# One more round of expert work in the first pass: the first expert starts on one tile in plain f32, the second on two

## The chip, the cores and the metric

The kernel runs on one core of a Trainium2 chip. The metric is the device time of one execution in microseconds (us). All times below come from one profiled execution of the kernel or from its timed runs.

## The reference

Three stages follow one another: attention that keeps only the 32 largest scores of each row, a mixture of eight experts whose gates are balanced by eight rounds of row and column normalisation, and a dense two-layer network. There are 2 x 576 = 1152 tokens of width 512.

```python
scores = scale * np.matmul(q, k.transpose(0, 1, 3, 2))          # q, k, v: (2, 8, 576, 64)
mask = scores >= kth                                             # the 32 largest of 576 stay
attn = exp(scores - max) * mask / (sum + 1e-9)
x = (attn @ v) as (1152, 512)

P = np.exp(x @ w_gate - max)                                     # (1152, 8)
for _ in range(8):
    P /= P.sum(1, keepdims=True) + 1e-09
    P /= P.sum(0, keepdims=True) + 1e-09
    P *= N / E
for e in range(8):                                               # w1[e]: (512, 1024), w2[e]: (1024, 512)
    out += P[:, e:e + 1] * (np.maximum(x @ w1[e], 0.0) @ w2[e])

h = out @ w_in                                                   # (512, 2048)
g = h * np.tanh(log1p(exp(h)))
return g @ w_out                                                 # (2048, 512)
```

## The kernel before, in words

**Tiles and chunks.** The 1152 tokens are nine tiles of 128. An expert's 1024 hidden columns are eight chunks of 128, numbered `f`. A chunk has an up part (`up`, line 622: weights stationary, tokens moving) and a down part (`down`, line 637: hidden tile stationary, 512 columns of weights moving). Both run in the split form: weights, tokens and hidden values are each a high and a low half of type f32r, and three products (high by high, high by low, low by high) replace one. An up part is 4 x 3 matmuls whose columns are the tokens. A down part is three matmuls of 512 columns for each tile. A tile and an expert together are the unit of work here: 9 x 8 = 72 such pairs must be done.

**Splitting.** For every chunk SP loads 2 x 256 KB of weights into one of four slots of `w_raw` (`load_slot`, lines 389 and 390), ScalarE copies them to `w_hi` (`split_hi`, line 898 through `copy`) and GpSimd subtracts to get `w_lo` (`split_lo`, line 1501). SP loads a slot again when `w_lo_done` says that GpSimd has read it. For hidden values ScalarE writes `h_f` and `ha_hi` (lines 970, 971) and GpSimd `ha_lo` (line 1508).

**Attention.** Nine tiles `T` of eight heads `h`. For each head TensorE transposes the masked probabilities of the head four back (line 514, and line 518 for the rest of a pair), computes the scores (504), and for every second head multiplies by the values in plain f32 (528, 533). VectorE finds the 32 largest scores in pairs of heads (1190, 1192), and masks from tile 3 on. In tiles 0 and 1 GpSimd masks (1532, 1535), in tile 2 it masks every second head. The next tile's queries are loaded by `next_queries` (381, 382), copied by ScalarE (`queries_high`, at the fourth head of the tile before), lowered by GpSimd and transposed by TensorE (493). A finished tile of attention is scaled with `row_sums` on VectorE (1199, 1201), transposed by `x_transposed` (541), and copied to `x_f`, `x_hi`, `x_lo`.

**First pass (`a`).** One expert chunk is put behind each head, `LAG = 5` heads into a tile. It begins at head 5 of tile 2. Its rounds are: expert 0 for tiles 0 and 1, experts 1 to 7 for tiles 0 to 2, and, as a ninth round, expert 0 again for tiles 2 to 4. So its 72 chunks hold 2 + 21 + 3 = 26 pairs. Results of the experts 0 to 6 go to DRAM (`spill`) and come back later; the last two are added by `add_last_a` (lines 1337 and 1341) while the second pass is on its first expert. Logits and the normalisation of the gates run between chunks behind attention.

**Second pass (`bc`).** For each expert the tiles that are left: expert 0 the tiles 5 to 8, the others the tiles 3 to 8, so 4 + 42 = 46 pairs. Its hidden values are copied high by ScalarE and low by VectorE (1302, 1311) out of PSUM. Expert 0 has one unit of 512 columns in each chunk with two banks in turn, the others two units of 384. The wait that frees a bank asks for the low half two units back:

```python
pe.wait_ge(hb_lo, units_bc(e, f) + j - 1 + TWO)
```

In program order TensorE does `up(f + 1)` before `down(f)`. The last stage (lines 846, 868) is the dense network; in its first half a chunk is two units of 320 columns and five tiles.

**Orders written by hand.** Each engine's order is fixed. On SP the queries of tile 2 are asked for before the first eight weight loads, which wait until all keys have left `w_raw`. On GpSimd each `chunk_a` is a `hidden_low` followed by the split of the chunk two ahead:

```python
chunk_a(*chunk_at(2, 7))
mask(2, 5)
chunk_a(*chunk_at(3, 0))
chunk_a(*chunk_at(3, 1))
mask(2, 7)
```

Of the kernel before, what the change touches and what calls it, by code (L numbers as in the profile page):

```python
# [11 lines left out]
def build(nc, q, k, v, w_gate, w1, w2, w_in, w_out, spill, out):  # L12
# [12 lines left out]
    DM = H * D  # L25
# [32 lines left out]
    NA = E + 1  # L58
    FIRST = 2
    LAST_UP = FIRST + BLK  # L60
    REST_BC = NT - LAST_UP

    def part_a(e):

        if isinstance(e, int) and e == 0:
            return 0, FIRST
        return (FIRST, BLK) if isinstance(e, int) and e == NA - 1 else (0, BLK)

    def weights_a(e):
        return e % E if isinstance(e, int) else e  # L70

    ctx = ExitStack()
    with ctx:
# [77 lines left out]
        w_hi_done, w_lo_done, w_used = sem("w_hi_done"), sem("w_lo_done"), sem("w_used")  # L151
        wg_split, lg_ready, lg_copied, gate_step = sem("wg_split"), sem("lg_ready"), sem("lg_copied"), sem("gate_step")
# [58 lines left out]
        def chunk_at(T, h):  # L211

            e, f = (T - MIX + 1, h + NF - LAG) if h < LAG else (T - MIX + 2, h - LAG)
            return (None, None) if isinstance(T, int) and e < 0 else (e, f)

        def new_x(e, f):

            return isinstance(e, int) and e < 2 and f == 0

        AFTER = (NT - MIX + 1) * NF + H + 4 - LAG  # L220
# [61 lines left out]
        A0, BC0 = 0, NA * NF  # L282
# [9 lines left out]
        FIRST_BANKS = (1, 3)  # L292

        def first_hidden(t, f):

            return t[:, 2 * (f % 2):2 * (f % 2) + 2, :].rearrange("p b n -> p (b n)")[:, 0:REST_BC * P]

        def fills(step0, e, f):

            return step0 // RING + e * (NF // RING) + f // RING + 1  # L300
# [63 lines left out]
        def _(sp):  # L364
# [31 lines left out]
            def first_of(e):  # L396
                return FIRST if isinstance(e, int) and e == 0 else BLK

            def load_ahead(e, queries=lambda: None):

                for f in range(NF):
# [3 lines left out]
                    if f == RING + 1:  # L405
                        sp.wait_ge(ya_copied, e + 1)
                        n = first_of(e)
                        sp.dma_start(spill[e, :, 0:n * DM],
                                     y_out[:, 0:n, :].rearrange("p t n -> p (t n)")).then_inc(y_spilled, 16)
# [20 lines left out]
            for f in range(RING, NF):  # L430
                load_experts(A0, 0, f)
            load_ahead(0, lambda: next_queries(MIX, (0, TB * P), (1, TB * P)))
            with sp.Fori(MIX, NT - 1) as T:
                load_ahead(T - MIX + 1, lambda: next_queries(T + 1, (1, (T - MIX) * P), (1, (T - MIX) * P + REST)))
            with sp.Fori(NT - MIX, E - 1) as e:
                load_ahead(e)
            for f in range(NF):
                load_experts(A0, NA - 1, f)
            sp.wait_ge(y_spilled, 16 * SPILLED)

            def expert_bc(e):
# [4 lines left out]
                n = first_of(e)  # L446
# [3 lines left out]
            with sp.Fori(1, SPILLED) as e:  # L450
# [25 lines left out]
        def _(pe):  # L476
# [141 lines left out]
            def up(s, first_tile, tiles, bank, ready, small=iter(())):  # L618

                terms = [(wt, xt, c) for c in range(DC) for wt, xt in ((w_hi, x_hi), (w_hi, x_lo), (w_lo, x_hi))]  # L620
                for n, (wt, xt, c) in enumerate(terms):
                    last = nc.tensor.matmul(ps[:, bank, 0:tiles * P], wt[:, s, 0, c * P:(c + 1) * P],  # L622
                                            xt[:, c, first_tile * P:(first_tile + tiles) * P],
# [5 lines left out]
            def down(s, hidden, slots, tiles, bank, first, final, bank_read, small=iter(()), after=None):  # L629

                hi, lo = hidden
                for t in range(tiles):
                    if first:
                        bank_read(t)
                    hs, r = slots[t // BLK], (t % BLK) * P
# [991 lines left out]
```

## Time and profile before

| what | value |
|---|---|
| median of 3 runs | 1291.96 us (1289.42 to 1293.16) |
| the profiled execution's own time | 1292.42 us |
| its span, first to last instruction | 1290.6 us |
| busy in the span: TensorE, VectorE, ScalarE, GpSimd | 1233.8, 768.4, 643.7, 508.3 us |
| mean granted clock of TensorE | 0.977 |
| chain that ended last, TensorE's share | 81% |

PE is the matmul part of TensorE, DVE is VectorE, ACT is ScalarE, POOL is GpSimd and SP issues the DMAs. A timeline row gives start, duration, engine, line, operation and tiles; in brackets stands the idle time before it and what ended it. A row of a stretch gives start:end, length, then busy time (and instructions) of PE, of PE's weight loads, of DVE, ACT and POOL, then TensorE's granted clock, the DMA share and GB/s. A chain row gives start, duration and what the end of the program hung on at that time. Plain f32 matmuls appear as two records each, so a count of 16 is 8 matmuls.

### The profile page before, as it was taken

What the parts mean: (1) busy time and instruction counts of PE and PEld (TensorE: products, weight loads), DVE (VectorE), ACT (ScalarE), POOL (GpSimd) and SP (SyncE); (2) the same over time, 40 slices, a digit from 0 to 9 for tenths busy, and PEclk for the clock granted to TensorE, in tenths of its full rate; (3) what the DMA queues carried; (4) which work ended last, traced back from release to release, by engine and by line L of the source; (5) the groups of instructions that cost most, each with busy time, mean ns of one, the idle gap of its engine ahead of it and who ended that gap; (6) DMA issues with size and microseconds to landing.
All of it is one profiled execution on the core that took longest, in us unless ns stands there. A gap on an engine that the chain in (4) does not pass through costs nothing.

```text
span 1290.6 us, 19241 instructions
## 1 busy us (share of the span) xinstructions
PE 1233.8 (96%) x6803; PEld 1105.8 (86%) x6803; DVE 768.4 (60%) x1376; ACT 643.7 (50%) x1162; POOL 508.3 (39%) x297
## 2 busy tenths in 40 slices
PE   4777899999999999999999999999999998999998
PEld 4666889999999999988998889999888998898776
DVE  6999898899999920554222131313131327877776
ACT  4766676677767753432222222222222226887775
POOL 1867765555656577754222222222222220000000
PEclk8877999999999999999999999999999999999999
DMA  9021332233323333332222121221313221222330
GB/s 163 9 66 58 90 99 91 91 114 91 106 89 107 107 99 118 119 126 86 91 66 89 54 84 65 71 84 46 107 33 106 66 66 49 67 82 67 97 123 33
DMA packets 145106, 108.91 MB, mean 84 GB/s; under 512 B 34576, under 2 KB 120592, under 8 KB 145040
## 3 DMA queue, kind: packets, MB, share of 16 engines
q1 hardware_dynamic: 145040, 108.05, 27.2%
q8 instruction: 39, 0.64, 0.2%
q14 instruction: 27, 0.22, 0.1%
HBM read 100.42 MB, written 7.60 MB: 84 GB/s over the span
## 4 chain that ended last, share of the span: by engine, by line
PE 81%; DVE 7%; ACT 6%; POOL 3%; issue 2%; DMA 0%; SPq 0%; POOLq 0%; DVEq 0%; ACTq 0%
PE ps L622 31%; PE ps L637 31%; PE ps L533 4%; PE ps L868 3%; PE ps L846 3%; PE ps L504 3%; PE ps L514 2%; DVE work L1192 2%; DVE top L1190 2%; ACT m_d L1121 1%; ACT m_r L1124 1%; PE ps L493 1%; POOL s_sb L1532 1%; ACT m_a L1119 1%; ACT m_r L1126 1%
## 5 line engine op out<-in xcount | busy, mean ns | idle before, releaser
L1501 POOL TENSOR_TENSOR w_lo<-w_raw,w_hi 128x1024 fp32r<-128x1024 f32 x138 | 333.1, 2414 | 410.3 <-ACT w_hi L898 410.3
L622 PE MATMUL ps<-x_hi,w_hi 128*128 128x384 f32 (+2 forms) x768 | 260.3, 339 | 0.1
L622 PE MATMUL ps<-x_hi,w_lo 128*128 128x384 f32 (+2 forms) x768 | 259.8, 338 | 0.0
L622 PE MATMUL ps<-x_lo,w_hi 128*128 128x384 f32 (+2 forms) x768 | 258.9, 337 | 0.0
L1311 DVE SCALAR_TENSOR_TENSOR h_lo<-ps,h_hi 128x384 fp32r<-128x384 f32 x112 | 62.2, 557 | 327.5 <-ACT h_hi L1094 327.5
L1094 ACT ACTIVATE h_hi<-ps 128x384 fp32r<-128x384 f32 x112 | 55.1, 492 | 358.3 <-PE ps L622 358.3
L898 ACT ACTIVATE w_hi<-w_raw 128x1024 fp32r<-128x1024 f32 (+1 forms) x172 | 179.5, 1044 | 0.5 <-DMA w_raw<-in_k 0.5
L1190 DVE MAX8 top<-work 128x8 f32<-128x576 f32 x216 | 152.3, 746 | 0.0
L622 PEld LDWEIGHTS ps<-x_hi,w_hi 128*128 128x128 f32 x768 | 144.6, 188 | 4.8 <-issue 0.3
L622 PEld LDWEIGHTS ps<-x_lo,w_hi 128*128 128x128 f32 x768 | 144.7, 188 | 3.9
L637 PE MATMUL ps<-w_hi,h_hi 128*128 128x512 f32 x368 | 146.1, 397 | 0.0
L622 PEld LDWEIGHTS ps<-x_hi,w_lo 128*128 128x128 f32 x768 | 144.4, 188 | 1.2
L637 PE MATMUL ps<-w_lo,h_hi 128*128 128x512 f32 x368 | 145.1, 394 | 0.0
L637 PE MATMUL ps<-w_hi,h_lo 128*128 128x512 f32 x368 | 145.1, 394 | 0.0
L1508 POOL TENSOR_TENSOR ha_lo<-h_f,ha_hi 128x384 fp32r<-128x384 f32 (+1 forms) x72 | 71.6, 994 | 100.5 <-ACT ha_hi L971 100.4
L1192 DVE MATCH_REPLACE8 work<-top,work 128x576 f32<-128x576 f32 x144 | 105.8, 742 | 0.0
L637 PE MATMUL ps<-w_hi,ha_hi 128*128 128x512 f32 x208 | 86.1, 414 | 0.0
L637 PEld LDWEIGHTS ps<-w_hi,h_lo 128*128 128x128 f32 x368 | 69.0, 188 | 17.1
L637 PE MATMUL ps<-w_hi,ha_lo 128*128 128x512 f32 x208 | 82.9, 398 | 0.0
L637 PE MATMUL ps<-w_lo,ha_hi 128*128 128x512 f32 x208 | 82.4, 396 | 0.0
L637 PEld LDWEIGHTS ps<-w_lo,h_hi 128*128 128x128 f32 x368 | 69.0, 187 | 14.2
L637 PEld LDWEIGHTS ps<-w_hi,h_hi 128*128 128x128 f32 x368 | 69.0, 188 | 13.9
(130 smaller groups left out, 2265.4 us busy)
## 6 DMA issues: line engine op xcount, KB each, us to landing
w_raw<-in_moe_w SPq DMA_DIRECT2D x272, 256.0 KB, 3.0
w_raw<-in_moe_w_in SPq DMA_DIRECT2D x32, 256.0 KB, 2.8
w_raw<-in_moe_w_out SPq DMA_DIRECT2D x32, 256.0 KB, 3.1
spill<-y_out SPq DMA_DIRECT2D x6, 768.0 KB, 3.8
y_in<-spill SPq DMA_DIRECT2D x6, 768.0 KB, 4.3
q_parts<-in_q SPq DMA_DIRECT2D x18, 128.0 KB, 3.2
vones<-in_v SPq DMA_DIRECT2D x8, 256.0 KB, 4.9
out<-acc SPq DMA_DIRECT2D x8, 256.0 KB, 2.9
```

The lines of the kernel that those rows point to most:

```text
L504: last = nc.tensor.matmul(ps[0:r + n, S_BANK + j, 0:HALF], q_s[:, part, h, 0:r + n], k_s[:, b, h // 2, (h % 2 * 2 + j) * HALF:(h % 2 * 2 + ...
L533: last = nc.tensor.matmul(ps[r:r + n, O_BANK, O_COL + a * DV:O_COL + (a + 1) * DV], pT[:, a, c, r:r + n], vones[:, b, c, h - 1 + a, :], st ...
L622: last = nc.tensor.matmul(ps[:, bank, 0:tiles * P], wt[:, s, 0, c * P:(c + 1) * P], xt[:, c, first_tile * P:(first_tile + tiles) * P], sta ...
L637: last = nc.tensor.matmul(ps[:, bank + t, 0:DM], ht[:, hs, r:r + P], wt[:, s, 1, :], start=(first and n == 0), stop=(final and n == 2))
L846: last = nc.tensor.matmul(ps[:, h2_bank(u), 0:w], wt[:, F % RING, 0, c * P:(c + 1) * P], xt[:, c, token:token + w], start=(n == 0), stop=( ...
L898: return nc.scalar.activation(dst, src, ACT.Copy)
L1094: nc.scalar.activation(h_hi[:, 2 * (f % 2) + j, :], ps[:, HB_BANK + j, 0:BT], ACT.Relu).then_inc(hb_relu, 1)
L1190: last = v_.max(top[:, b, op // 2, :], src)
L1192: last = v_.match_replace(work[:, par, :], top[:, b, op // 2, :], src, LOWEST)
L1311: v_.scalar_tensor_tensor(out=h_lo[:, s, :], in0=ps[:, HB_BANK + j, 0:BT], scalar=0.0, in1=h_hi[:, s, :], op0=ALU.max, op1=ALU.subtract).t ...
L1501: g_.tensor_tensor(w_lo[:, s, :, :].rearrange("p a n -> p (a n)"), w_raw[:, s, :, :].rearrange("p a n -> p (a n)"), w_hi[:, s, :, :].rearr ...
L1508: g_.tensor_tensor(ha_lo[:, f % 2, 0:w], h_f[:, f % 2, 0:w], ha_hi[:, f % 2, 0:w], ALU.subtract).then_inc(ha_split, 1)
```

## The change

The first pass gets a tenth round (`NA = E + 2`) and starts eight heads earlier, at head 5 of tile 1. Round 0 is expert 0 for tile 0 alone, in plain f32: four f32 matmuls of 128 columns up and one f32 matmul of 512 columns down in each chunk, straight from `w_raw`, without a split; SP reloads its slots on the new count `first_used`. Round 1 is expert 1 for tiles 0 and 1. Rounds 2 to 7 are the experts 2 to 7 for three tiles. Rounds 8 and 9 do expert 0 for tiles 1 to 3 and expert 1 for tiles 2 to 4. The second pass then has five tiles for expert 0 (two units of 320 columns), four for expert 1 (one unit of 512, two banks in turn), and six for the others: 27 + 45 = 72 pairs. On SP the queries of tile 2 are asked for behind the first eight weight loads. On GpSimd the splits of steps 0 and 1 move from ahead of tile 2's first mask to behind it, and those of steps 4 to 6 each move past a mask. `add_last_a` has nine additions and not six. On TensorE the transposition of tile 1 of x waits for the eighth f32 hidden tile.

```diff
-    NA = E + 1
-    FIRST = 2
+    NA = E + 2
+    LATE_A = (1, 2)
...
         def units_bc(e, f):
-            return f if isinstance(e, int) and e == 0 else 2 * (e * NF + f) - NF
+            if isinstance(e, int) and e == 1:
+                return 2 * NF + f
+            return 2 * f if isinstance(e, int) and e == 0 else 2 * (e * NF + f) - NF
...
+        def parts_bc(e, f):
+            if isinstance(e, int) and e == 1:
+                return [(1 + f % 2, 0, 4 * P)]
+            w = (2 * BLK - skip_bc(e)) * P // 2
+            bank = 1 if isinstance(e, int) and e == 0 else HB_BANK
+            return [(bank, 0, w), (bank + 1, w, w)]
...
             next_queries(1, (0, P), (0, P + REST))
-            next_queries(2, (0, 2 * P), (0, 2 * P + REST))
             sp.wait_ge(k_low0, KC)
             sp.wait_ge(k_low1, KC)
             for f in range(RING):
-                load_experts(A0, 0, f)
+                load_first(f)
+            next_queries(2, (0, 2 * P), (0, 2 * P + REST))
+            for f in range(RING, NF):
+                sp.wait_ge(first_used, f - RING + 1)
+                load_first(f)
             next_queries(3, (0, 3 * P), (0, 3 * P + REST))
...
             def x_transposed(T):
                 pe.wait_ge(xn_done, 2 * T + 2)
+                if isinstance(T, int) and T == 1:
+                    pe.wait_ge(ha_relu, NF + FREE)
...
+            def up_first(f):
+                pe.wait_ge(raw_in[f % RING], 32 * (f // RING + 1))
+                pe.wait_ge(ha_relu, f + FREE)
+                if f == 0:
+                    pe.wait_ge(x_copied, 1)
+                for c in range(DC):
+                    last = nc.tensor.matmul(ps[:, X_BANK, 0:P], w_raw[:, f % RING, 0, c * P:(c + 1) * P], x_f[:, c, :],
+                                            start=(c == 0), stop=(c == DC - 1))
+                last.then_inc(ha_ready, 1)
+
+            def down_first(f):
+                pe.wait_ge(ha_relu, f + 1 + FREE)
+                nc.tensor.matmul(ps[:, YA_BANK, 0:DM], h_f[:, f % 2, 0:P], w_raw[:, f % RING, 1, :],
+                                 start=(f == 0), stop=(f == NF - 1)).then_inc(first_used, 1)
...
-                dve.wait_ge(ya_added, 2 * BLK)
-                for t in range(BLK):
-                    v_.scalar_tensor_tensor(out=acc[:, FIRST + t, :], in0=m_a[:, t, :],
-                                            scalar=gate[:, FIRST + t, 0:1], in1=acc[:, FIRST + t, :],
-                                            op0=ALU.mult, op1=ALU.add).then_inc(ya_added, 1)
+                for e, y in enumerate((m_d, m_a)):
+                    dve.wait_ge(ya_added, (2 + e) * BLK)
+                    for t in range(BLK):
+                        to = LATE_A[e] + t
+                        v_.scalar_tensor_tensor(out=acc[:, to, :], in0=y[:, t, :], scalar=gate[:, to, e:e + 1],
+                                                in1=acc[:, to, :], op0=ALU.mult, op1=ALU.add).then_inc(ya_added, 1)
...
-            pool.wait_ge(k_tr, 4 * KC)
-            for f in range(AHEAD):
-                split_lo(A0 + f, f % RING)
             normalised(1, 0)
             normalised(1, 1)
             mask(2, 1)
             queries_low(3)
+            split_lo(0, 0)
             x_low(1)
+            split_lo(1, 1)
             chunk_a(*chunk_at(2, 5))
             mask(2, 3)
             chunk_a(*chunk_at(2, 6))
-            chunk_a(*chunk_at(2, 7))
+            hidden_low(*chunk_at(2, 7))
             mask(2, 5)
-            chunk_a(*chunk_at(3, 0))
-            chunk_a(*chunk_at(3, 1))
+            split_lo(4, 0)
+            hidden_low(*chunk_at(3, 0))
+            split_lo(5, 1)
+            hidden_low(*chunk_at(3, 1))
             mask(2, 7)
+            split_lo(6, 2)
```

## Rows read from the trace of the kernel before

**Rows 1.** The page: busy tenths of the 40 slices of the span.

```profile
PE   4777899999999999999999999999999998999998
...
DVE  6999898899999920554222131313131327877776
```

**Rows 2.** Busy time by stretch: start:end, length, engines, granted clock, DMA.

```profile
72.39:114.52 42.13, 30.89 (x169) 27.63 (x169) 40.71 (x86) 24.87 (x54) 30.68 (x21) 0.69 0.11 32
114.52:165.05 50.53, 44.16 (x298) 40.55 (x299) 45.26 (x89) 34.12 (x73) 36.32 (x25) 0.92 0.23 69
165.05:562.62 397.57, 396.73 (x2488) 365.26 (x2486) 311.85 (x575) 253.96 (x476) 249.53 (x156) 1.00 0.32 104
...
606.19:1066.70 460.51, 460.51 (x2310) 415.52 (x2310) 115.79 (x170) 106.11 (x165) 133.33 (x56) 1.00 0.23 73
```

**Rows 3.** The chain in the second pass: start, us, what.

```profile
582.64 2.73 PE ps L622 x12
585.37 2.79 PE ps L637 x12
...
610.36 4.19 PE ps L637 x18
614.56 4.19 PE ps L622 x24
```

**Rows 4.** The chain in the last stage, 320 columns up, five tiles down.

```profile
1131.88 3.52 PE ps L846 x24
1135.39 3.50 PE ps L868 x15
```

**Rows 5.** The chain in the third tile: plain f32 work.

```profile
157.25 0.22 PE ps L528 x2
...
167.93 1.73 PE ps L533 x16
```

**Rows 6.** Busy time and granted clock in pieces of 5 us.

```profile
115.00:120.00 5.00, 5.00 (x29) 4.76 (x29) 5.00 (x11) 3.31 (x8) 1.94 (x2) 0.62 0.01 3
120.00:125.00 5.00, 5.00 (x41) 4.88 (x41) 5.00 (x10) 3.37 (x8) 2.24 (x2) 1.00 0.00 0
```

**Rows 7.** ScalarE's timeline: tile 2's queries, and scores of tile 1's head 5.

```profile
67.17 1.14 ACT L898 ACTIVATE q_parts<-q_parts 128x512 fp32r<-128x512 f32 x2
...
74.01 0.69 ACT L898 ACTIVATE s_sb<-ps 128x576 f32<-128x576 f32 x1
```

**Rows 8.** The DMA queue's timeline: queries, then weights.

```profile
55.49 0.60 SPq L381 DMA_DIRECT2D q_parts<-in_q  x1
...
67.74 0.51 SPq L390 DMA_DIRECT2D w_raw<-in_moe_w  x1
```

**Rows 9.** The landing of those eight weight loads.

```profile
DMA to landing us min/median/max: 2.9/4.3/5.5
```

**Rows 10.** VectorE's timeline: a pair begun, and two waits for attention output.

```profile
78.24 1.41 DVE L1190 MAX8 top<-s_sb 128x8 f32<-128x576 f32 x2
...
109.69 0.17 DVE L1199 TENSOR_SCALAR rsum<-o_sb 128x4 f32<-128x4 f32 x1 [1.35 <-ACT o_sb L898]
...
159.60 0.17 DVE L1199 TENSOR_SCALAR rsum<-o_sb 128x4 f32<-128x4 f32 x1 [4.89 <-ACT o_sb L898]
```

**Rows 11.** GpSimd's timeline: the weight split ahead of a mask.

```profile
148.89 2.41 POOL L1501 TENSOR_TENSOR w_lo<-w_raw,w_hi 128x1024 fp32r<-128x1024 f32 x1 [2.09 <-ACT w_hi L898]
```

**Rows 12.** TensorE's timeline where two heads of the fourth tile begin.

```profile
142.41 0.63 PE L514 MATMUL ps<-ident,e_sb 128*128 128x128 f32 x4 [1.40 <-issue]
...
154.53 0.66 PE L514 MATMUL ps<-ident,e_sb 128*128 128x128 f32 x4 [1.80 <-POOL e_sb L1535]
```

**Rows 13.** VectorE's timeline around the six additions.

```profile
581.19 4.21 DVE L1337 SCALAR_TENSOR_TENSOR acc<-y_out,gate,acc 128x512 f32<-128x512 f32 x3
...
587.42 0.68 DVE L1302 SCALAR_TENSOR_TENSOR h_lo<-ps,h_hi 128x512 fp32r<-128x512 f32 x1
```

**Rows 14.** GpSimd's timeline beside them.

```profile
581.50 2.68 POOL L1501 TENSOR_TENSOR w_lo<-w_raw,w_hi 128x1024 fp32r<-128x1024 f32 x1 [3.36 <-ACT w_hi L898]
```

More of the change, by code:

```diff
@@ L394, in load_experts, with load_first, spill_out @@
                 load_weights(step0 + e * NF + f, s, w1_v[of, :, :, f * P:(f + 1) * P], w2[of, f * P:(f + 1) * P, :])
-            def first_of(e):
-                return FIRST if isinstance(e, int) and e == 0 else BLK
+            def load_first(f):
+                load_slot(f % RING, w1_v[0, :, :, f * P:(f + 1) * P], w2[0, f * P:(f + 1) * P, :])
+            def spill_out(e):
+                sp.wait_ge(ya_copied, e + 1)
+                n = part_a(e)[1]
+                sp.dma_start(spill[e, :, 0:n * DM],
+                             y_out[:, 0:n, :].rearrange("p t n -> p (t n)")).then_inc(y_spilled, 16)
             def load_ahead(e, queries=lambda: None):
@@ L405, in load_ahead @@
                     if f == RING + 1:
[L406 to L409, printed above, removed]
+                        spill_out(e)
             def next_queries(T, low, high):
@@ L627, in up, with down @@
                     next(small, None)
-            def down(s, hidden, slots, tiles, bank, first, final, bank_read, small=iter(()), after=None):
+            def down(s, hidden, tiles, bank, first, final, bank_read, small=iter(()), after=None):
                 hi, lo = hidden
@@ L764, in expert_pass @@
                     down_chunk(0, f)
-                with pe.Fori(1, E - 1) as e:
+                for f in range(NF):
+                    up_chunk(1 + (f + 1) // NF, (f + 1) % NF)
+                    down_chunk(1, f)
+                with pe.Fori(2, E - 1) as e:
                     for f in range(NF):
@@ L979, in expert_a_copied @@
             def expert_a_copied(e):
-                act.wait_ge(w_used, e * NF + RING)
-                n = FIRST if isinstance(e, int) and e == 1 else BLK
-                if isinstance(e, int) and e == NA:
-                    copy(m_a[:, 0:n, :], ps[:, YA_BANK:YA_BANK + n, :]).then_inc(ya_copied, 1)
+                if isinstance(e, int) and e == 1:
+                    act.wait_ge(first_used, NF)
+                else:
+                    act.wait_ge(w_used, (e - 1) * NF + RING)
+                n = part_a(e - 1)[1]
+                if isinstance(e, int) and e > E:
+                    to = m_d if e == E + 1 else m_a
+                    copy(to[:, 0:n, :], ps[:, YA_BANK:YA_BANK + n, :]).then_inc(ya_copied, 1)
                     return
@@ L1288, in add_expert @@
                 dve.wait_ge(w_used, done + RING)
-                skip = LAST_UP - BLK if isinstance(e, int) and e == 0 else 0
+                skip = skip_bc(e)
                 for t in range(skip, 2 * BLK):
@@ L1355, in _ @@
             expert_bc(1)
-            with dve.Fori(2, E) as e:
+            expert_bc(2)
+            with dve.Fori(3, E) as e:
                 expert_bc(e)
@@ L1560, in _ @@
                 mask(1, h)
-            pool.wait_ge(k_tr, 4 * KC)
-            for f in range(AHEAD):
-                split_lo(A0 + f, f % RING)
             normalised(1, 0)
```

156 lines of the change are left out of this document (81 added, 75 removed).

## The prediction

> **What bounds the kernel now.** I read the busy digits of the page first, then the busy time by stretch, then the chain, and last the timelines of single engines. The digits say that TensorE is full from the sixth slice on, while VectorE is full until slice 14 and then mostly idle [rows 1]. The stretches sharpen this. From 165.05 us (tile 3, head 5) to 562.62 TensorE is busy for 396.73 of 397.57 us, and in the second pass for every microsecond, at full clock; from 72.39 to 114.52 us, where the new f32 round would run, it is busy for 30.89 of 42.13 us at a mean clock of 0.69 while VectorE is busy for 40.71; from 114.52 to 165.05 it is idle for 6.4 us [rows 2]. So behind 165 us the time is TensorE's work, and ahead of it the time is set by VectorE's search and what it waits for. Two things count: how much TensorE work leaves the full stretch, and whether head 5 of tile 3 comes earlier or later.
>
> **Second pass: what leaves.** A unit of 12 matmuls of 512 columns takes 2.73 us, four tiles down (12 matmuls) 2.79, two units of 384 columns (24) 4.19, six tiles down (18) 4.19 [rows 3]. Two units of 320 columns take 3.52 and five tiles down (15) 3.50, in the last stage, by the same instruction forms [rows 4]. Expert 0 now costs 2.73 + 2.79 = 5.52 us a chunk and will cost 3.52 + 3.50 = 7.02: 8 x 1.50 = +12.0. Expert 1 costs 4.19 + 4.19 = 8.38 and will cost 5.52: 8 x 2.86 = -22.9. Together -10.9 us. The first pass keeps eight two-tile chunks and 64 three-tile chunks behind head 5 of tile 2, so nothing else changes in TensorE's full stretch. Extra loads (16 of 256 KB) meet an idle queue: the DMA share is 0.11 in the early stretch [rows 2].
>
> **First stretch: what comes.** No row shows a plain f32 matmul of 128 or 512 columns. The nearest are 8 of 65 columns (16 records) in 1.73 us, 0.216 each, and one of 130 columns (2 records) in 0.22 us [rows 5]. Twice the columns cost nothing more, so the short one is bound by something fixed (loading its weights fits) and the price of 128 columns is 0.22. For 512 columns, below: as cheap per column as the longer row, 512/130 x 0.22 = 0.87 us; above: at half clock, 1.74. A chunk is 4 x 0.22 + 0.87 = 1.75 us at full clock, 3.5 at half. Eight are 14 us or 28 us, against 42.13 - 30.89 = 11.2 us of idle time. The clock decides. In 115 to 120 us TensorE was busy all the time at a mean of 0.62, and in the 5 us behind it, still busy, it had full clock [rows 6]: work without gaps brought the clock from 1.2 to 2.4 GHz. The new work fills just the gaps, and 30.89 us at a mean clock of 0.69 are only some 21 us at full clock (an estimate, busy time by mean clock). 21 + 14 = 35 of 42 us fits. I take full clock for most of it; both ends go into the range.
>
> **The queries of tile 2.** This is the term that the diff hides. They are asked for at 55.49 us now, and ScalarE begins on them at 67.17 [rows 7, 8]. Moved behind the eight weight loads, the last of which is issued at 67.74 [rows 8], they are issued at 68.3 and 68.9 and queue behind 2 MB whose last load lands up to 5.5 us after its issue [rows 9], at about 73.2. ScalarE works in order, so it stands from 67.17 to about 73.2, 6.0 us, with the key copies, the next scores and probabilities of heads 4 and 5 queued behind it. Head 5's scores, copied at 74.01 to 74.70 now [rows 7], come 6.0 us later, at 80.7; VectorE begins its search on heads 4 and 5 at 78.24 and wants the second head's 0.7 us later [rows 10], so it is 1.8 us late. In heads 6 and 7 and in tile 2's heads 0 and 1 `up_first` stands in TensorE's order between the scores and the query transposition whose copy the next head waits for, 0.9 us each; I count another 1 to 2 us. Of the two the search gets back some 1.4 us, its present wait for attention's last pair at head 3 [rows 10], because that product ran at half clock. I take VectorE 2 us late at tile 2, head 4 (0.6 to 3.2).
>
> **The two masks.** On GpSimd the split at 148.89 stood ahead of a mask that TensorE then waited for 1.80 us at 154.53, and a like one cost 1.40 at 142.41 [rows 11, 12]. VectorE in turn stood 4.89 us at 159.60 for that head's attention [rows 10]. With splits 4 to 6 behind the masks, both masks come 4 us earlier and TensorE runs through: -3.2 us. Against it stand the 2 us from above and 0.4 us more, because GpSimd now does the splits of steps 0 and 1 (2.4 us each) between tile 2's first mask and its third. Head 5 of tile 3 comes 0.8 us earlier: -0.8 (bounds -3 and +6).
>
> **The nine additions.** `add_last_a` runs behind VectorE's low half of chunk 4, and the low half of chunk 5 is queued behind it. Now six additions run from 581.19 to 587.42; the first three take 4.21 us because GpSimd's split of 581.50 gets between them, the other three 2.0, so an addition is 0.67 us and the wait 2.2 [rows 13, 14]. The low half at 587.42 [rows 13] was in time, because with one unit a chunk and two banks `up(6)` needs only the low half of `up(4)`. With two units of 320 on two banks it needs that of `up(5)`. Let 0 be the end of `up(4)`: TensorE does down(3), up(5), down(4), so up(6) may start at 3.50 + 3.52 + 3.50 = 10.5. Additions began 1.3 us behind the end of `up(4)` at 579.85 (582.64 less one down part of 2.79, rows 3), with the shorter unit 1.0; nine are 6.0, one wait 2.2, so the last begins at 8.5 and all end at 9.2: in time by a little, with half a microsecond for the low half. But GpSimd's next split falls due 1.6 us behind the end of `up(5)` (581.50 less 579.85), a little less with the shorter unit, and that is 8.5 as well. If it gets in ahead of the ninth addition, that one ends near 11.7, the low half at 12.2, and TensorE waits 1.7 us. A tie; I take the middle, +0.9 (bounds 0 and 2.6, the latter if the split gets in an addition earlier and holds up two low halves).
>
> By the Trainium skill, SBUF — State Buffer, section "SBUF: two separate sides", an addition with two SBUF inputs and a GpSimd operation that reads SBUF exclude each other for a whole instruction, whichever starts first. The stretched first three additions agree. Read strictly, the sum changes by the tie alone: +1.7 if the split starts first, 0 if the addition does.
>
> Nothing else is on the path: unrolled loops met no idle time before; the round copied to `m_d` replaces a spill of the same size.
>
> **The sum.** -10.9 - 0.8 + 0.9 = -10.8 us. The profiled span of 1290.6 becomes 1279.8, its own time of 1292.4 becomes 1281.6. That execution lies 0.5 us over the median of 1291.96, so the median becomes 1281.2 (-0.8%). No change can be told from one within 0.3%, 3.9 us.
>
> **Rivals.**
> - More is gained (0.18). Full clock throughout takes 3 us more out of the first stretch, as the 30.89 busy us there are 21 at full clock: 1275.5 to 1278.
> - The early lateness is kept (0.15). ScalarE's 6.0 us go through to tile 3 with nothing made good: -10.9 + 0.9 + 6.0 = -4.0, 1288.0. For it: VectorE is busy 40.71 of 42.13 us and has no reserve [rows 2]. Against it: the search works on a pair of heads at a time and has its scores before it begins.
> - Slower (0.07). The f32 round runs at half clock: 28 us into 11.2 us of gaps is +16.8, less the masks' 3.2, so +13.6 - 10.9 + 0.9 = +3.6, 1295.6, and a little over that with the bound of the additions, 1297.3. It decides when the first stretch loses over 10 us, that is when most of the round sees half clock. Against it: gapless work regained full clock [rows 6]. By TensorE: Matmul & The Clock Gate (the Trainium skill, Part 1) half rate is the default state and activity releases it; that is this rival's mechanism read either way, and the row behind 120 us [rows 6] agrees with the release.
>
> **How the numbers follow.** My forecast has 0.60 and its own range is 1278 to 1285. With the rivals, eight in ten lie in 1276 to 1289. Faster by over 0.3% (below 1288.1): 0.60 + 0.18 + half of the 0.15, 0.85. Slower (above 1295.8): 0.05. Within: the rest, 0.10.
>
> **What would show it.** Right: ScalarE idle about 6 us ahead of the tile-2 queries; f32 pairs of records at 0.22 and 0.87 us; no wait for masks around 142 and 154 us; 7.0 us a chunk for expert 0 and 5.5 for expert 1; at most one TensorE wait, of about 1.7 us, before `up(6)` of expert 0. It would be wrong if the granted clock stayed near a half up to 115 us, or if head 5 of tile 3 came over 6 us late.

## The result and the profile after

The changed kernel takes 1279.74 us (median of six runs, 1279.32 to 1281.27), the kernel before beside it 1292.56 us (six runs, 1288.23 to 1294.66). The ratio is 0.9909, interval 0.9891 to 0.9926: 11.8 us faster, 9.6 to 14.1. The forecast was a median of 1281.2 us and faster. The profiled execution took 1280.16 us with a span of 1278.0, 12.6 us less than before. The runs also lie closer together, within 2.0 us instead of 6.4.

The page's digits, as in [rows 1], with the granted clock below:

```profile
PE   4768999999999999999999999999999998999998
...
DVE  6989998899999930455222222213131317887776
...
PEclk8789999999999999999999999999999999999999
```

TensorE is full from the fifth slice on, one earlier than before. The busy time by stretch shows the same at finer grain (columns as in [rows 2]); the stretches are cut at the start of the f32 round's first matmul (85.04), at tile 2's head 4 (113.48), at tile 3's head 5 (162.2), and around the second pass:

```profile
67.34:85.04 17.70, 8.60 (x57) 7.81 (x55) 13.67 (x29) 8.50 (x19) 9.95 (x8) 0.71 0.39 103
85.04:113.48 28.44, 26.77 (x196) 21.89 (x195) 27.85 (x61) 18.38 (x46) 17.29 (x13) 1.00 0.34 103
113.48:162.20 48.72, 44.77 (x322) 40.26 (x323) 47.41 (x96) 37.67 (x80) 44.34 (x30) 1.00 0.42 130
162.20:559.70 397.50, 396.63 (x2499) 366.11 (x2498) 312.57 (x576) 254.45 (x478) 248.87 (x156) 1.00 0.32 102
609.38:1054.00 444.62, 444.62 (x2202) 397.47 (x2201) 109.41 (x161) 104.99 (x160) 134.47 (x57) 1.00 0.24 76
```

In the stretch of the f32 round TensorE is now busy for 26.77 of 28.44 us at full clock; in [rows 2] the stretch from 72.39 to 114.52 us had a mean of 0.69. Head 5 of tile 3 begins at 162.22 us, which was 165.05. From there to the end of the first pass nothing changed (397.5 us), and then comes the second pass.

**The early part.** ScalarE's and VectorE's timelines, beside [rows 7, 10]:

```profile
75.79 1.15 ACT L947 ACTIVATE q_parts<-q_parts 128x512 fp32r<-128x512 f32 x2 [8.45 <-DMA q_parts<-in_q]
```

```profile
83.13 0.76 DVE L1246 MAX8 top<-s_sb 128x8 f32<-128x576 f32 x1 [3.33 <-ACT s_sb L947]
...
112.29 0.20 DVE L1255 TENSOR_SCALAR rsum<-o_sb 128x4 f32<-128x4 f32 x1 [0.52 <-ACT o_sb L947]
...
156.77 0.17 DVE L1255 TENSOR_SCALAR rsum<-o_sb 128x4 f32<-128x4 f32 x1 [1.24 <-ACT o_sb L947]
```

ScalarE began on tile 2's queries at 75.79 us where it was 67.17, after 8.45 us of waiting for their load. VectorE then waited 3.33 us for head 5's scores. The wait for attention's output at head 3 shrank from 1.35 to 0.52 us, the one in tile 3 from 4.89 to 1.24. The f32 instructions, from TensorE's timeline (two records for each matmul, ends overlap) and the price of a down part from the chain:

```profile
87.75 1.05 PE L681 MATMUL ps<-x_f,w_raw 128*128 128x128 f32 x8
...
89.08 1.02 PE L687 MATMUL ps<-w_raw,h_f 128*128 128x512 f32 x2
```

```profile
121.72 0.91 PE ps L687 x2
```

From 87.75 to the next instruction at 88.64 the four up matmuls take 0.89 us, a down part 0.91. In the kernel before TensorE waited for a mask of tile 2 three times: at head 7 of tile 2, in this row of its timeline, and at the two places of [rows 12].

```profile
129.19 1.09 PE L514 MATMUL ps<-ident,e_sb 128*128 128x128 f32 x4 [3.07 <-issue]
```

In the changed kernel the two waits of [rows 12] are gone. The first is left, 1 us shorter, and so is the wait for a copy of ScalarE behind head 5 of tile 3, which was 0.76 us at 167.05 before:

```profile
131.47 0.63 PE L540 MATMUL ps<-ident,e_sb 128*128 128x128 f32 x4 [2.09 <-issue]
...
164.23 0.65 PE L519 MATMUL ps<-ident,q_parts 128*128 128x128 f32 x4 [0.77 <-ACT p_rest L947]
```

**The second pass.** The chain, as in [rows 3, 4]: expert 0's down and up parts, then expert 1's.

```profile
598.88 3.50 PE ps L664 x15
602.38 3.52 PE ps L650 x24
...
609.38 2.73 PE ps L650 x12
```

```profile
618.34 2.79 PE ps L664 x12
```

These are 7.02 us a chunk for expert 0 and 5.52 for expert 1. VectorE's and GpSimd's timelines around the nine additions, beside [rows 13, 14], and what TensorE waited for from 170 us on:

```profile
584.00 4.21 DVE L1386 SCALAR_TENSOR_TENSOR acc<-y_out,gate,acc 128x512 f32<-128x512 f32 x3
588.25 2.08 DVE L1392 SCALAR_TENSOR_TENSOR acc<-m_d,gate,acc 128x512 f32<-128x512 f32 x3
590.36 4.21 DVE L1392 SCALAR_TENSOR_TENSOR acc<-m_a,gate,acc 128x512 f32<-128x512 f32 x3
594.50 0.88 DVE L1359 SCALAR_TENSOR_TENSOR h_lo<-ps,h_hi 128x320 fp32r<-128x320 f32 x2
```

```profile
584.59 2.42 POOL L1553 TENSOR_TENSOR w_lo<-w_raw,w_hi 128x1024 fp32r<-128x1024 f32 x1 [4.84 <-ACT w_hi L947]
591.61 2.41 POOL L1553 TENSOR_TENSOR w_lo<-w_raw,w_hi 128x1024 fp32r<-128x1024 f32 x1 [4.61 <-ACT w_hi L947]
```

```profile
PE ps L650 <- DVE h_lo L1359: 1.5, 1, 1.5
```

GpSimd's second split started at 591.61, during the eighth addition by the starts and lengths shown, and so ahead of the ninth. The last three additions took 4.21 us like the first three, and TensorE stood for 1.5 us before `up(6)`. From 170 us to the last stage that is its one wait.

The accounts, by fixed places in the two traces. The transposition of tile 2 of x, the last thing ahead of head 5 of tile 3, begins at 164.62 before and 161.78 after: -2.84. The first transposition of the last stage begins at 1066.92 and 1054.93: -11.99, so -9.15 between, which is the 1.5 us wait and -10.65 for the chunks. The last stage gave 0.6 more, up to -12.6. All of it lies behind the start of the last down part (6.8 us to the end before, 6.2 after), where the last results are copied and stored. The last stage takes 223.7 to 224.1 us in the traces of the kernel before and its variants, 223.0 to 223.2 in those of the changed kernel and its variants. What makes this is not shown.

### The profile page after: what moved, and what is told of

It is laid out like the page before. It is cut to its first block, busy times and chain, and to the rows that moved or that the text cites. A ratio compares the mean times of both kernels' runs of the same rounds, so it can differ in the third digit from the quotient of the medians.

```text
span 1278.0 us, 19203 instructions
## 1 busy us (share of the span) xinstructions
PE 1225.9 (96%) x6859; PEld 1095.8 (86%) x6859; DVE 766.4 (60%) x1376; ACT 643.7 (50%) x1171; POOL 507.8 (40%) x297
## 4 chain that ended last, share of the span: by engine, by line
PE 80%; DVE 8%; ACT 7%; POOL 2%; issue 2%; DMA 1%; SPq 0%; DVEq 0%; ACTq 0%; POOLq 0%
PE ps L650 31%; PE ps L664 31%; PE ps L559 4%; PE ps L917 4%; PE ps L895 3%; PE ps L530 3%; PE ps L540 2%; DVE work L1248 1%; ACT m_d L1177 1%; DVE top L1246 1%; ACT m_r L1180 1%; PE ps L519 1%; ACT m_a L1175 1%; ACT m_r L1182 1%; DVE m_r L1442 1%
## 5 line engine op out<-in xcount | busy, mean ns | idle before, releaser
L1553 POOL TENSOR_TENSOR w_lo<-w_raw,w_hi 128x1024 fp32r<-128x1024 f32 x138 | 332.3, 2408 | 397.5 <-ACT w_hi L947 397.4
L1359 DVE SCALAR_TENSOR_TENSOR h_lo<-ps,h_hi 128x384 fp32r<-128x384 f32 (+2 forms) x120 | 66.6, 557 | 338.3 <-ACT h_hi L1143 338.3
L650 PE MATMUL ps<-x_hi,w_hi 128*128 128x384 f32 (+3 forms) x768 | 258.7, 337 | 1.6 <-DVE h_lo L1359 1.5
L650 PE MATMUL ps<-x_hi,w_lo 128*128 128x384 f32 (+3 forms) x768 | 257.9, 336 | 0.0
L650 PE MATMUL ps<-x_lo,w_hi 128*128 128x384 f32 (+3 forms) x768 | 257.0, 335 | 0.0
L1143 ACT ACTIVATE h_hi<-ps 128x384 fp32r<-128x384 f32 (+2 forms) x120 | 59.0, 491 | 377.0 <-PE ps L650 377.0
L664 PE MATMUL ps<-w_hi,h_hi 128*128 128x512 f32 x360 | 142.9, 397 | 0.0
L664 PE MATMUL ps<-w_lo,h_hi 128*128 128x512 f32 x360 | 142.0, 394 | 0.0
L664 PE MATMUL ps<-w_hi,h_lo 128*128 128x512 f32 x360 | 141.9, 394 | 0.0
```

The source lines that it names most:

```text
L650: last = nc.tensor.matmul(ps[:, bank, 0:w], wt[:, s, 0, c * P:(c + 1) * P], xt[:, c, token:token + w], start=(n == 0), stop=(n == len(term ...
L664: last = nc.tensor.matmul(ps[:, bank + t, 0:DM], ht(t * P), wt[:, s, 1, :], start=(first and n == 0), stop=(final and n == 2))
L1143: nc.scalar.activation(hidden_bc(h_hi, f, at, w), ps[:, bank, 0:w], ACT.Relu).then_inc(hb_relu, 1)
L1359: v_.scalar_tensor_tensor(out=hidden_bc(h_lo, f, at, w), in0=ps[:, bank, 0:w], scalar=0.0, in1=hidden_bc(h_hi, f, at, w), op0=ALU.max, op1 ...
L1553: g_.tensor_tensor(w_lo[:, s, :, :].rearrange("p a n -> p (a n)"), w_raw[:, s, :, :].rearrange("p a n -> p (a n)"), w_hi[:, s, :, :].rearr ...
```

## The experiments

All marks are of one trace each; "x(0)" and "x(2)" are the starts of the transpositions of tiles 0 and 2 of x. The ratio is to the kernel before in the same session; its median there was 1292.56 (changed kernel), 1293.03 (experiments 1 to 3 and the thin round of 4), 1291.9 (masks alone, both, queries first with the thin round, queries late) or 1292.86 us (the last four rows), so medians of different sessions compare to about 1 us.

| kernel | median, range (us) | ratio, 95% interval | x(0) | x(2) | span |
|---|---|---|---|---|---|
| before | 1292.56, 1288.2 to 1294.7 | | 69.76 | 164.62 | 1290.6 |
| after | 1279.74, 1279.3 to 1281.3 | 0.9909, 0.9891 to 0.9926 | 69.84 | 161.78 | 1278.0 |
| queries first | 1277.26, 1276.1 to 1278.3 | 0.9884, 0.9865 to 0.9902 | 69.98 | 159.35 | 1275.6 |
| splits back | 1284.43, 1283.4 to 1285.7 | 0.9941, 0.9923 to 0.9960 | 70.21 | 165.49 | 1281.7 |
| additions parted | 1278.26, 1277.4 to 1278.7 | 0.9891, 0.9873 to 0.9909 | 70.23 | 161.54 | 1276.2 |
| thin f32 round | 1281.47, 1279.3 to 1283.1 | 0.9916, 0.9890 to 0.9942 | 70.96 | 161.74 | 1279.4 |
| masks alone | 1291.99, 1287.7 to 1294.8 | 1.0000, 0.9987 to 1.0012 | 69.57 | 160.87 | 1288.3 |
| queries first, additions parted | 1275.30, 1274.2 to 1276.4 | 0.9882, 0.9867 to 0.9897 | 69.76 | 157.55 | 1272.0 |
| queries first, thin round | 1280.81, 1276.6 to 1281.1 | 0.9922, 0.9907 to 0.9937 | 69.95 | 157.36 | 1274.4 |
| queries late alone | 1295.11, 1292.6 to 1298.2 | 1.0034, 1.0020 to 1.0048 | 69.84 | 164.64 | 1290.8 |
| filler | 1289.90, 1288.2 to 1290.9 | 0.9980, 0.9971 to 0.9988 | 69.80 | 160.50 | 1286.9 |
| filler, masks | 1287.54, 1286.0 to 1289.2 | 0.9967, 0.9952 to 0.9981 | 69.85 | 158.52 | 1285.8 |
| before, once more | 1295.21 (one run) | | 72.16 | 167.06 | 1293.4 |
| masks alone, once more | 1288.44 (one run) | | 71.80 | 158.99 | 1286.6 |

### 1. The queries asked for first, in the changed kernel

```diff
             next_queries(1, (0, P), (0, P + REST))
+            next_queries(2, (0, 2 * P), (0, 2 * P + REST))
...
-            next_queries(2, (0, 2 * P), (0, 2 * P + REST))
             for f in range(RING, NF):
                 sp.wait_ge(first_used, f - RING + 1)
```

> The changed kernel with the queries of tile 2 asked for before the first weight loads again. My account: ScalarE's 8.45 us of waiting for them and VectorE's 3.3 us at 83 us vanish, TensorE still fits the f32 round between 72 and 114 us, and head 5 of tile 3, at 162.2 us in the changed kernel, comes at 159 to 160.5: the span goes from 1278.0 to about 1275.5 (1274.5 to 1276.5). Rival: the wait was absorbed, as TensorE with the f32 round is the limit of that stretch anyway; then head 5 of tile 3 stays within 1 us of 162.2 and the span within 1 us of 1278.

Faster by 2.5 us, and no run of either kernel lies in the other's range. Its busy time by stretch:

```profile
72.00:85.00 13.00, 9.05 (x71) 7.76 (x72) 13.00 (x28) 8.19 (x20) 8.65 (x7) 1.00 0.03 12
85.00:114.00 29.00, 26.03 (x185) 21.02 (x183) 28.40 (x62) 18.87 (x44) 18.87 (x14) 1.00 0.39 121
```

VectorE is busy for all 13 us from 72 to 85 and the f32 round still fits: 26.03 of 29 us at full clock. The transposition of tile 2 of x comes 2.4 us earlier. My account held; the rival, that TensorE limits the stretch anyway, fell. By VectorE's masking for tile 2's head 4 the queries cost more than 2.5 us: it begins at 108.60 here (the first row) and at 112.62 in the changed kernel (the second), 4.0 later. This trace then lost 1.5 us again, because it had half clock at head 7 of tile 2 (the third row), where the changed kernel's had full clock (the table of experiment 5).

```profile
108.60 0.80 DVE L1242 SCALAR_TENSOR_TENSOR e_sb<-s_sb,top,e_sb 128x576 f32<-128x576 f32 x1
```

```profile
112.62 0.80 DVE L1242 SCALAR_TENSOR_TENSOR e_sb<-s_sb,top,e_sb 128x576 f32<-128x576 f32 x1
```

```profile
127.60 1.09 PE L540 MATMUL ps<-ident,e_sb 128*128 128x128 f32 x4 [2.25 <-issue]
```

### 2. The splits back ahead of the masks, in the changed kernel

```diff
             hidden_low(*chunk_at(2, 7))
+            split_lo(4, 0)
             mask(2, 5)
-            split_lo(4, 0)
             hidden_low(*chunk_at(3, 0))
             split_lo(5, 1)
             hidden_low(*chunk_at(3, 1))
+            split_lo(6, 2)
             mask(2, 7)
-            split_lo(6, 2)
```

> The changed kernel with GpSimd's splits of steps 4 and 6 ahead of the two masks of tile 2 again. If the masks' place gave what I counted, TensorE waits for masks again near 139 and 150 us, 3.2 us together, and the span is 1281.2; as the changed trace gained 5.1 us between head 7 of tile 2 and head 5 of tile 3, up to 5 us is possible (1283). Rival: those waits came from something else (the half clock there, or the late chain of hidden values), and the span stays within 1 us of 1278.

4.7 us slower by the medians, 3.7 by the spans (1281.7), inside the expected 1281.2 to 1283. TensorE's two waits are back at once, with the sizes of [rows 12]:

```profile
143.27 0.63 PE L540 MATMUL ps<-ident,e_sb 128*128 128x128 f32 x4 [1.41 <-issue]
...
155.41 0.66 PE L540 MATMUL ps<-ident,e_sb 128*128 128x128 f32 x4 [1.82 <-POOL e_sb L1587]
```

### 3. The nine additions in two parts, in the changed kernel

Six stay behind the low half of chunk 4, three (from `m_a`) go behind that of chunk 5.

```diff
-                if i == ITERS:
-                    add_last_a()
+                if i in (ITERS, ITERS + 1):
+                    add_last_a(i - ITERS)
```

> The changed kernel with the nine additions in two parts, six behind the low half of chunk 4 and three behind that of chunk 5 of the second pass's first expert. My account: the one wait of TensorE for VectorE's low half, 1.5 us before the up part of chunk 6, vanishes: span 1276.5. Rival: the wait hangs on the clash with GpSimd's split wherever the additions stand, and comes again at the next chunk: span 1278.

1.5 us faster, as expected. What TensorE waited for from 500 to 900 us is an empty list:

```profile
core 0 of [0], span 1276.2 us
engine line waited for: us in total, times, longest us
```

### 4. Most of the f32 round left out, with the change's order and with the queries first

One matmul of 128 columns up and one of 128 columns down replace four of 128 and one of 512, so tile 0's part of expert 0 is missing from the output.

```diff
-                for c in range(DC):
-                    last = nc.tensor.matmul(ps[:, X_BANK, 0:P], w_raw[:, f % RING, 0, c * P:(c + 1) * P], x_f[:, c, :],
-                                            start=(c == 0), stop=(c == DC - 1))
+                last = nc.tensor.matmul(ps[:, X_BANK, 0:P], w_raw[:, f % RING, 0, 0:P], x_f[:, 0, :],
+                                        start=True, stop=True)
...
-                nc.tensor.matmul(ps[:, YA_BANK, 0:DM], h_f[:, f % 2, 0:P], w_raw[:, f % RING, 1, :],
+                nc.tensor.matmul(ps[:, YA_BANK, 0:P], h_f[:, f % 2, 0:P], w_raw[:, f % RING, 1, 0:P],
```

> The changed kernel with most of the f32 round's matmuls left out: one of 128 columns up and one of 128 columns down in each chunk in place of four of 128 and one of 512, so expert 0's result for tile 0 is missing. Tells what the f32 work costs in its place. My account (it lies in gaps): the granted clock between 85 and 113 us falls again below 0.8 and head 5 of tile 3 comes at 161 to 162.5. Rival (the round is paid in full or in part, hidden by the masks' gain): head 5 of tile 3 comes at 155 to 159 and the span is under 1275.

> The thin f32 round (one matmul of 128 columns up and one of 128 down in each chunk, expert 0's result for tile 0 is missing) with the queries of tile 2 asked for first. Beside the run with the queries first and the full round it tells what the f32 work costs once nothing else delays the stretch. If it lies in gaps: within 1 us of that run. If TensorE is the limit there: head 5 of tile 3 comes 2 us or more earlier.

With the change's order the mark x(2) comes at 161.74 instead of 161.78. With the queries first VectorE's masking for tile 2's head 4 begins at 108.56 instead of 108.60, but x(2) comes at 157.36 instead of 159.35. That is the 2 us which I had named as the sign that TensorE is the limit. 1.5 of it are the half clock at head 7 in the trace of experiment 1; against experiment 9, which has the full f32 round and full clock there, x(2) is 0.2 us earlier. Head 7 of tile 2 comes at 127.06, at 127.60 in experiment 1. So the f32 work costs at most some 0.5 us where it stands. My guess on the clock was wrong for that trace. It stayed at full there and was 0.97 behind:

```profile
85.04:113.48 28.44, 19.54 (x154) 17.52 (x153) 28.09 (x61) 18.82 (x46) 17.28 (x13) 1.00 0.36 108
113.48:162.20 48.72, 43.71 (x317) 40.34 (x316) 47.23 (x96) 36.11 (x77) 43.18 (x29) 0.97 0.41 128
```

What I had not expected is that doing less was slower: 1281.47 against 1279.74, with overlapping ranges, and with the queries first 1280.81 against 1277.26, from different sessions, where the two ratio intervals do not overlap (0.9907 to 0.9937, 0.9865 to 0.9902). The first trace shows where its span lost 1.4 us, and it isn't the clock of the f32 round. TensorE waits 1.3 us longer at the first place behind x(2) (0.77 in the changed kernel), because the queries of tile 4 landed later (see experiment 5):

```profile
165.50 0.66 PE L519 MATMUL ps<-ident,q_parts 128*128 128x128 f32 x4 [2.08 <-ACT p_rest L946]
```

With the queries first this wait is 1.64 us, 0.85 in experiment 1. That trace was taken in its shortest run (1276.58; the other three took 1280.7 to 1281.1), so it doesn't show what the other three lost. I took the loss for the clock's, which led to the fillers below; for the thin round itself that is not shown.

### 5. The masks' place alone, in the kernel before

```diff
-            chunk_a(*chunk_at(2, 7))
+            hidden_low(*chunk_at(2, 7))
             mask(2, 5)
-            chunk_a(*chunk_at(3, 0))
-            chunk_a(*chunk_at(3, 1))
+            split_lo(4, 0)
+            hidden_low(*chunk_at(3, 0))
+            split_lo(5, 1)
+            hidden_low(*chunk_at(3, 1))
             mask(2, 7)
+            split_lo(6, 2)
```

> The kernel before with one part of the change alone: GpSimd's splits of steps 4 to 6 each behind the next mask of tile 2. My account: the waits of 1.40 us at 142 and 1.80 us at 154 go, head 5 of tile 3 comes at about 161.8 instead of 165.05, and the span is 1287.4 (-3.2). Rival: the f32 round's denser TensorE work, through the clock, was what gained, and the masks alone give under 1 us.

> The kernel before with the splits behind the masks, for a second trace. The first had head 5 of tile 3 at 161.3 us, 3.7 us earlier than in the kernel before, of which 1.05 us went again at the next head, while eleven runs gave no gain. If the first trace was a lucky one, head 5 comes at 163 to 167 here, with half clock between 115 and 160 us; if not, at 161.3.

Eleven runs gave 1.0000, so under 1.7 us of gain by the interval. Its first trace has the mark x(2) 3.75 us earlier, and gives 1.05 us of it back at the next head, where TensorE waits for ScalarE:

```profile
164.37 0.66 PE L493 MATMUL ps<-ident,q_parts 128*128 128x128 f32 x4 [1.82 <-ACT p_rest L898]
```

ScalarE had stood 1.29 us for the queries of tile 4 and was busy from then on, with the copies of x in line behind them:

```profile
157.11 1.15 ACT L898 ACTIVATE q_parts<-q_parts 128x512 fp32r<-128x512 f32 x2 [1.29 <-DMA q_parts<-in_q]
```

In all nine traces with the masks moved ScalarE waits for this load (0.23 to 1.58 us), and TensorE's row above follows 7.25 to 7.26 us behind the end of that wait. In the five others ScalarE doesn't wait for it. So the load of tile 4's queries is the next limit behind the masks. No run asked for it earlier.

The clock explains the rest of what the traces disagree on. At head 7 of tile 2, behind the first wait for a mask, the four transpositions take 1.09 us in five traces (half clock) and 0.63 in nine (full clock). From their start to x(2) the fourteen traces show four lengths:

| head 7 of tile 2 to x(2), us | half clock at head 7 | full clock at head 7 |
|---|---|---|
| splits ahead of the masks | 35.43, 35.44 (before, both traces) | 33.94 (splits back), 33.95 (queries late), 33.95 (filler) |
| masks ahead of the splits | 31.75 (queries first), 31.82 (masks alone), 31.89 (filler, masks) | 30.30 to 30.33 (after and five more) |

So the masks' place gives 3.6 us at either clock, in the kernel before as in the changed one, and the half clock costs 1.5 us with either order. In the kernel before 1.05 of the 3.6 us go again to tile 4's queries.

The second trace had full clock at head 7: from x(0) to x(2) it takes 87.2 us, the first 91.3, the kernel before 94.9 in both of its traces. Both traces show a gain of 2.5 us or more at the end of the second pass, and the timed runs show none. The first was taken in a run of 1290.10 us, 1.9 under the median of its eleven, which is part of the difference. The rest is not settled.

### 6. The queries late alone, in the kernel before

```diff
             next_queries(1, (0, P), (0, P + REST))
-            next_queries(2, (0, 2 * P), (0, 2 * P + REST))
...
             for f in range(RING):
                 load_experts(A0, 0, f)
+            next_queries(2, (0, 2 * P), (0, 2 * P + REST))
             next_queries(3, (0, 3 * P), (0, 3 * P + REST))
```

> The kernel before with one part of the change alone: the queries of tile 2 asked for behind the first eight weight loads. My account: ScalarE waits for them about 8.4 us, VectorE about 4 us at 79 to 83 us, and as the stretch there is VectorE's, head 5 of tile 3 comes 2.5 to 4 us later: span 1293 to 1294.5. Rival (absorbed): within 1 us of 1290.6.

Slower by 0.34% (0.20 to 0.48), 2.6 to 6.2 us, for an expected 2.4 to 3.9 (1293 to 1294.5 against 1290.6), with VectorE's wait at the same place and of the same size as in the changed kernel:

```profile
82.98 0.76 DVE L1190 MAX8 top<-s_sb 128x8 f32<-128x576 f32 x1 [3.35 <-ACT s_sb L898]
```

Its trace was taken in its shortest run and has x(2) at 164.64, no later than before: what it lost by tile 2 (115.67 instead of 112.73 for the transposition of tile 1 of x) it had again by tile 3. At head 7 it was 1.5 us late (130.69 for 129.19), and there this trace had full clock and the kernel before half clock, which is worth the same 1.5 us. The price comes from the timed runs and from experiment 1, not from that trace.

### 7. Filler matmuls in the kernel before

Four plain f32 matmuls of 128 columns, ones by the identity into a bank that nobody reads, twice a head from head 5 of tile 1 to head 4 of tile 2. They take the f32 round's time and places and do nothing else.

```diff
+            def fill(T, h):
+                if isinstance(T, int) and (1, 5) <= (T, h) <= (2, 4):
+                    for _ in range(4):
+                        nc.tensor.matmul(ps[:, YA_BANK, 0:P], ones[:, :], ident[:, :], start=True, stop=True)
...
                     scores(T, h, parts)
+                    fill(T, h)
...
+                    fill(T, h)
                     if expert is not None:
                         down_before(expert, f)
```

> The kernel before with idle work added and nothing else: eight plain f32 matmuls of 128 columns, ones by the identity into an unused bank, with each head from head 5 of tile 1 to head 4 of tile 2, as much TensorE time as the f32 round takes there (14 us in all) and in its two places. Theory (leaving the f32 work out cost 2 to 4 us, so it pays through the clock): the granted clock from 85 to 114 us goes from 0.73 to over 0.95, the kernel becomes 1 to 3 us faster than before (1289 to 1291) though it does 14 us more work, and its runs lie closer together than those of the kernel before, which spread over 6.7 us. Rival (the clock there doesn't matter): equal or up to 3 us slower, with the same spread.

> The same filler, and the splits of steps 4 to 6 behind the masks of tile 2. The masks' place alone gave nothing that the runs could tell (ratio 1.000), while its loss in the changed kernel cost 4.7 us. If the clock is what joins them: 3 to 5 us faster than the filler alone (1285 to 1287), with a narrow spread. If the masks pay only beside the rest of the change (expert 1's later splits): within 1 us of the filler alone.

The kernel before with 14 us of useless TensorE work is 0.20% faster (0.12 to 0.29), about 2.6 us, and its runs lie within 2.7 us, those of the kernel before beside it within 5.9. All three are as expected. Busy time and clock by stretch:

```profile
72.00:85.00 13.00, 10.05 (x76) 9.82 (x77) 13.00 (x28) 7.16 (x17) 8.65 (x7) 0.87 0.02 6
85.00:114.00 29.00, 26.90 (x229) 25.78 (x227) 28.93 (x62) 18.65 (x39) 23.06 (x16) 1.00 0.16 47
114.00:130.00 16.00, 12.67 (x100) 11.69 (x99) 16.00 (x33) 11.39 (x26) 11.16 (x8) 1.00 0.10 34
```

The same places in the kernel before:

```profile
85.00:114.00 29.00, 20.94 (x117) 18.67 (x117) 27.58 (x59) 17.30 (x37) 21.90 (x15) 0.73 0.16 47
114.00:130.00 16.00, 12.42 (x77) 11.52 (x78) 16.00 (x34) 10.06 (x21) 10.10 (x9) 0.82 0.10 34
```

From 85 to 114 us the clock is 1.00 where it was 0.73, from 114 to 130 it is 1.00 where it was 0.82, and x(2) comes at 160.50. Head 7 of tile 2 comes 2.6 us earlier (126.55 for 129.19), and full clock there gives the other 1.5. As the fillers compute nothing that is used, I see no other way to a gain than the clock. With the masks moved as well the ratio is 0.9967 (0.9952 to 0.9981). That is 1.7 us more by the ratios, half of what I had expected at the least, and the intervals of the two overlap. Their traces differ by 1.1 us (spans 1286.9 and 1285.8), and the marks say why: the masks gave 3.6, half clock at head 7 took 1.5, and the later wait for tile 4's queries 1.0.

### 8. The kernel before once more

> The kernel before, unchanged, for a second trace of it. Its runs spread from 1288 to 1295 us. If the granted clock makes the spread, this trace differs from the first in which stretches ahead of head 5 of tile 3 had half clock, and by as much in the time of that head (165.05 us in the first), and by nothing behind it.

This run took 1295.21 us, 2.8 more than the first profiled one. The first two stretches of the first trace and of this one:

```profile
0.00:50.00 50.00, 28.51 (x152) 25.58 (x153) 38.01 (x82) 28.21 (x56) 20.58 (x22) 0.80 0.63 106
50.00:72.00 22.00, 15.35 (x122) 13.53 (x121) 21.64 (x47) 17.54 (x39) 17.34 (x13) 1.00 0.35 105
```

```profile
0.00:50.00 50.00, 29.83 (x142) 26.88 (x142) 36.78 (x80) 28.02 (x54) 20.19 (x21) 0.73 0.60 106
50.00:72.00 22.00, 17.73 (x120) 16.58 (x120) 20.22 (x45) 15.36 (x35) 15.42 (x13) 0.84 0.28 79
```

The 2.4 us are all there by x(0) (72.16 against 69.76), and from x(0) to x(2) both traces take 94.9 us. The difference lies in the first 72 us, where the clock differs too, earlier than I had said. Whether the clock made it or fell with it is not shown.

### 9. The best version

> The changed kernel with the queries of tile 2 asked for first and the nine additions in two parts. If both are independent, the span is 1278.0 - 2.5 - 1.5 = 1274.0. If the queries' wait was absorbed, 1276.5.

Queries first and additions parted: 1275.30 us, ratio 0.9882 (0.9867 to 0.9897), the fastest kernel here, 4.4 us under the changed one by the medians, 3.5 by the ratios, as they were measured in different sessions. Its ratio is that of experiment 1 within the interval. Its trace has the shortest span, 1272.0, where 1274.0 was expected: the queries are worth 4.0 us at tile 2's head 4 (masking at 108.38, 112.35 in experiment 3), and experiment 1's trace had shown only 2.5 because of its half clock at head 7.

## Why the prediction was right, step by step

- **The second pass, -10.9.** Right in form and size: 7.02 and 5.52 us a chunk as summed, -10.65 us by the marks.
- **The f32 round in the gaps.** Right. 0.89 and 0.91 us at full clock for 0.88 and 0.87, the clock rose as said, and leaving three quarters of the work out moved x(2) by 0.0 and 0.2 us between traces of the same clock at head 7. It was undersized in one way: I took gapless work as free, but it pays. The filler, with no useful result, gave 2.6 us to the old kernel.
- **The queries, with what attention gave back at head 3.** Right mechanism, a little too small: VectorE 2.6 us late at tile 2's head 4 (masking at 112.62, 109.99 before) for a forecast of 2. ScalarE waited 8.45 us, not 6.0. The last load of weights was taken to land at 73.2 and the queries with it; ScalarE could begin on them at 75.8, 6.4 us behind their second issue. The queries alone cost 4.0 us (112.62 against 108.60 in experiment 1), for 1.8 and a further 1 to 2. The 1.4 us given back came as forecast (109.99 against 108.60).
- **From there to head 7.** -0.35 us (19.20 before, 18.85 after), where the splits of steps 0 and 1 were to cost 0.4. That cost did not appear.
- **The two masks.** Right, 3.6 us for 3.2, as experiments 2 and 5 show.
- **The clock at head 7.** This step was missing from the sum. The old trace has half clock there, the new one full clock, and that is 1.5 us by the table of experiment 5. Together with the masks it makes the 5.1 us between head 7 of tile 2 and head 5 of tile 3 (35.9 before, 30.8 after). It is in part luck: experiment 1, with the same f32 round ahead of it, had half clock at that head.
- **Early part, -0.8.** Mis-sized: -2.8, which is 2.6 - 0.35 - 3.6 - 1.5. The sum had 2.0 + 0.4 - 3.2. The largest error is the clock.
- **The additions, +0.9 for a tie.** The split got in, 1.5 us, against 1.7 for that case; parting the additions took it away whole. The +0.9 was the middle between two cases and not a time that could come out.
- **What cancelled and what did not.** The trace gained 12.6 us for a forecast of 10.8. The early part gave 2.0 more than the sum had, 1.5 of it by the clock at head 7. The rest cancelled nearly: the additions cost 0.6 us more than the sum had, the chunks of the second pass gave 0.25 less, and the last stage gave 0.6 that it had not.
- **The rivals.** "The early lateness is kept" was the nearest: it exists (2.5 us in experiment 1, 2.6 to 6.2 in experiment 6), but the rest of the stretch outweighed it. "More is gained" named full clock as its reason, and that came true for 1.5 of its 3 us. "Slower at half clock" found no support in any stretch of the f32 round.

## What to carry to other kernels

Moving work from a stretch where TensorE is full into one where it has gaps is worth its full price in the first, and can be worth more where the fuller stretch keeps the clock, as the fillers show here. Before an edit is judged by two traces, compare the granted clock at the places where it falls: here one place differed from trace to trace of like kernels and moved everything behind it by 1.5 us. Read where each DMA lands in the consumer's order before moving it behind a burst on the same queue: here one moved line cost a fifth of the change's gain. When a unit is cut in two on the same two banks, the wait reaches back half as far, and any run of work queued on the engine that frees the bank must become shorter with it.

## What the runs showed of the hardware

- Useless plain f32 matmuls made the kernel faster: 14 us of them, 0.20% (0.12 to 0.29), with the granted clock from 85 to 114 us at 1.00 instead of 0.73.
- The runs of the kernel before spread over 5.9 to 6.7 us in its four sessions (its variants without added TensorE work over 5.6 and 7.1). With the full f32 round the spread is 1.3 to 2.3 us, with the filler 2.7 and 3.2, with the thin round 3.8 and 4.5. Between two traces of the kernel before the difference lay in the first 72 us, with a clock of 0.84 or 1.00 from 50 to 72 us. That stretch lies ahead of the added work, so why the spread shrinks is not shown.
- At head 7 of tile 2 TensorE had half clock in five of fourteen traces and full clock in nine, worth 1.5 us. The length of the idle time just before does not sort them: half clock came behind 3.07, 3.08, 3.08, 2.25 and 1.98 us, full clock behind 1.73 to 2.28.
- A query load of two times 128 KB took 3.0 us from issue to landing in the kernel before and 6.5 us behind 2 MB of weights on the same queue (medians of its two parts).
